# Attention's packed values contracted on 32x32 tiles of the PE array, with the exponentials turned by VectorE in place of TensorE

## The reference

```python
def sm_attn(qq, kk, vv):
    s = scale * np.matmul(qq, kk.transpose(0, 1, 3, 2))
    s = s - np.max(s, axis=-1, keepdims=True)
    a = np.exp(s)
    a = a / (np.sum(a, axis=-1, keepdims=True) + 1e-09)
    return np.matmul(a, vv)
p_packed = sm_attn(p, k, v)             # 32 packed rows against 576 keys
out = sm_attn(q, p_packed, p_packed)    # 576 tokens against 32 packed rows
# x: out as 4608 tokens x 512
xn = x / rms(x) * rms_g
x = (silu(xn @ w_gate) * (xn @ w_val)) @ w_out      # 512 -> 1536 -> 512
x = ((x @ w1) * (x @ w2) @ w3) @ w_out2             # 512 -> 1024 -> 1024 -> 512
```

## Time and profile before

| what | value |
|---|---|
| median of 3 runs | 1412.69 us |
| lowest and highest | 1411.97 and 1413.43 us |
| the profiled execution's own time | 1412.07 us |
| its span in the trace | 1410.3 us |
| PE busy, share of the span | 1386.3 us, 98% |
| DVE busy | 605.7 us, 43% |
| ACT busy | 406.9 us, 29% |
| POOL busy | 141.4 us, 10% |

### The profile page before, as it was taken

One profiled execution on the slowest core, in us unless ns is written; L12 is line 12 of the kernel. 1 busy time (PEld: TensorE's weight loads), 2 busy tenths in 40 slices (PEclk: granted clock), 3 DMA queues, 4 the chain that ended last, 5 costly groups with the idle time before them and its releaser, 6 DMA issues.

```text
span 1410.3 us, 22634 instructions
## 1 busy us (share of the span) xinstructions
PE 1386.3 (98%) x9688; PEld 1194.8 (85%) x9688; DVE 605.7 (43%) x1095; ACT 406.9 (29%) x803; POOL 141.4 (10%) x137
## 2 busy tenths in 40 slices
PE   7989999999999999999999999999999999999999
PEld 5679899898898998988989988888888888888887
DVE  3657556565565565655655632212212111212111
ACT  4253342433423424334233422111111111111111
POOL 0100100001001000010012030220202020202000
PEclk9999999999999999999999999999999999999999
DMA  9882451533424515323024130101011010100000
GB/s 332 233 314 82 129 163 41 196 106 93 165 86 128 163 39 197 107 92 131 18 69 167 47 107 0 60 0 60 0 60 45 16 60 0 60 0 30 0 30 30
DMA packets 59155, 129.13 MB, mean 92 GB/s; under 512 B 3504, under 2 KB 12720, under 8 KB 57264
## 3 DMA queue, kind: packets, MB, share of 16 engines
q1 hardware_dynamic: 59056, 127.70, 27.6%
HBM read 106.69 MB, written 20.99 MB: 91 GB/s over the span
## 4 chain that ended last, share of the span: by engine, by line
PE 95%; DVE 3%; ACT 1%; issue 1%; DMA 0%; SPq 0%; DVEq 0%; ACTq 0%
PE psum L586 9%; PE psum L584 9%; PE psum L585 9%; PE psum L546 8%; PE psum L565 7%; PE psum L567 7%; PE psum L566 7%; PE psum L547 7%; PE psum L548 7%; PE psum L606 5%; PE psum L605 5%; PE psum L604 5%; PE psum L513 3%; PE psum L500 1%; PE psum L526 1%; PE psum L467 1%
## 5 line engine op out<-in xcount | busy, mean ns | idle before, releaser
L546 PE MATMUL psum<-a_hi,m_hi 128*128 128x288 f32 x768 | 240.7, 313 | 0.4
L565 PE MATMUL psum<-g_hh,wo_hi 128*128 128x288 f32 x768 | 227.4, 296 | 4.5 <-DVE g_res L921 2.6
L547 PE MATMUL psum<-a_lo,m_hi 128*128 128x288 f32 x768 | 226.7, 295 | 0.0
L548 PE MATMUL psum<-a_hi,m_lo 128*128 128x288 f32 x768 | 226.3, 295 | 0.0
L567 PE MATMUL psum<-g_hh,wo_lo 128*128 128x288 f32 x768 | 226.0, 294 | 0.0
L566 PE MATMUL psum<-g_hl,wo_hi 128*128 128x288 f32 x768 | 225.9, 294 | 0.0
L1012 DVE TENSOR_TENSOR b_h<-b_s,psum 128x512 f32<-128x512 f32 x72 | 49.5, 688 | 408.9 <-PE psum L586 408.9
L584 PE MATMUL psum<-xh,w_hi 128*128 128x512 f32 x576 | 224.1, 389 | 0.0
L585 PE MATMUL psum<-xl,w_hi 128*128 128x512 f32 x576 | 224.1, 389 | 0.0
L586 PE MATMUL psum<-xh,w_lo 128*128 128x512 f32 x576 | 224.1, 389 | 0.0
L546 PEld LDWEIGHTS psum<-a_hi,m_hi 128*128 128x128 f32 x768 | 144.4, 188 | 50.6 <-issue 46.6
(11 more groups left out here) (109 smaller groups left out, 1737.2 us busy)
## 6 DMA issues: line engine op xcount, KB each, us to landing
w_in<-in_w_gate SPq DMA_DIRECT2D x24, 1024.0 KB, 5.3
w_in<-in_w_val SPq DMA_DIRECT2D x24, 1024.0 KB, 5.3
kT<-in_kT SPq DMA_DIRECT2D x8, 1152.0 KB, 7.7
v_sb<-in_v SPq DMA_DIRECT2D x8, 1152.0 KB, 7.2
qT<-in_qT SPq DMA_DIRECT2D x16, 576.0 KB, 3.8
y_scratch<-g_res SPq DMA_DIRECT2D x16, 576.0 KB, 3.2
x_raw<-y_scratch SPq DMA_DIRECT2D x9, 1024.0 KB, 7.6
out<-b_res SPq DMA_DIRECT2D x8, 1024.0 KB, 5.2
```

Source lines behind the costliest of these rows:

```text
L546: nc.tensor.matmul(in_ps[which], hi, a2_hi[:, t, par, :], start=par == 0, stop=False)
L547: nc.tensor.matmul(in_ps[which], hi, a2_lo[:, t, par, :], start=False, stop=False)
L548: last = nc.tensor.matmul(in_ps[which], lo, a2_hi[:, t, par, :], start=False, stop=par == 1)
L565: nc.tensor.matmul(out_ps[m], hi, hh[:], start=f == 0, stop=False)
```

## The change

The exponentials are no longer turned by TensorE. VectorE turns them in 32x32 blocks, from `sc` to the new tile `e1T` (`turn1`, one instruction for each parity): the block of head c's 32 packed rows and 32 keys stays on partitions 32 c to 32 c + 31, with the keys now on the partitions. The items AT and ScalarE's copies after them are gone, and so is `a1T`.

PV now contracts over 32 keys at a time: 18 blocks x 2 parities x 4 heads = 144 calls, weights 32 keys x 32 packed rows, moving operand 32 keys x 64 dimensions. The row tile of head (c, par) is c, and its column tile is `packed(par, c)`: c for even heads and c + 2 (modulo 4) for odd ones. So the packed rows of odd heads stand two places on in `pp`, in S2 and in M; `rden1` of odd heads is written by two reciprocals that move partitions, and `g` is laid out to match. `v` is laid out in 128 partitions in place of 96, with as many bytes. `sums1` moves from slot (0, 3) to (0, 5), and `turn1` stands in (0, 3) and (0, 4).

```diff
-SLOT_ITEM = {(0, 1): ("M", 0, 4), (0, 2): ("M", 0, 5), (0, 3): ("AT", 1, 0), (0, 4): ("AT", 1, 1), (0, 5): ("PV", 1, 0),
+SLOT_ITEM = {(0, 1): ("M", 0, 4), (0, 2): ("M", 0, 5), (0, 5): ("PV", 1, 0),
...
+def packed(par, c):
+    place = (c + 2 * par) % HC
+    return slice(NP * place, NP * (place + 1))
...
-            v_sb = at("v_sb", [TP, 2, NT, HC * DH])
+            v_sb = at("v_sb", [P, 2, NB, DH])
-            a1T = at("a1T", [TP, 2, NT * P])
+            e1T = at("e1T", [P, 2, S])
...
-                if kind == "AT":
-                    pe.wait_ge(e1_ready, 2 * a + part + 1)
-                    for j in range(NT):
-                        last = nc.tensor.transpose(xy[j // 3][0:TP, j % 3 * P:(j % 3 + 1) * P], sc[:, part, TP * j:TP * (j + 1)], ident[:])
                 if kind == "PV":
-                    freed(pe, "AT", a, 1)
+                    pe.wait_ge(e1T_ready, 2 * (a + 1))
                     pe.wait_ge(v_loaded, 16 * (a + 1))
-                    for par in range(2):
-                        for j in range(NT):
+                    for j in range(NB):
+                        for par in range(2):
                             for c in range(HC):
-                                last = nc.tensor.matmul(xy[par][NP * c:NP * (c + 1), 0:DH], a1T[:, par, P * j + NP * c:P * j + NP * (c + 1)],
-                                                        v_sb[:, par, j, DH * c:DH * (c + 1)], start=j == 0, stop=j == NT - 1)
+                                rows = slice(NP * c, NP * (c + 1))
+                                last = nc.tensor.matmul(xy[par][packed(par, c), 0:DH], e1T[rows, par, NP * j:NP * (j + 1)],
+                                                        v_sb[rows, par, j, :], start=j == 0, stop=j == NB - 1)
...
-                            rows, cols = slice(DH * par, DH * (par + 1)), slice(NP * c, NP * (c + 1))
+                            rows, cols = slice(DH * par, DH * (par + 1)), packed(par, c)
...
                 if kind == "S1":
                     full(act, "S1", a, part)
+                    if a:
+                        act.wait_ge(e1T_ready, 2 * a)
...
-                if kind == "AT":
-                    full(act, "AT", a, part)
-                    nc.scalar.copy(a1T[:, part, :].rearrange("p (a n) -> p a n", a=2), psum[0:TP, 6:8, 0:3 * P]).then_inc(xy_free, 1)
...
-                nc.vector.reciprocal(rden1[:], den1[:]).then_inc(rden1_ready, 1)
+                nc.vector.reciprocal(rden1[:, 0:1], den1[:, 0:1])
+                nc.vector.reciprocal(rden1[DH:P, 1:2], den1[0:DH, 1:2])
+                nc.vector.reciprocal(rden1[0:DH, 1:2], den1[DH:P, 1:2]).then_inc(rden1_ready, 1)
+
+            def turn1(a, par):
+                dve.wait_ge(e1_ready, 2 * a + par + 1)
+                if a:
+                    full(dve, "PV", a - 1, 0)
+                nc.vector.transpose(e1T[:, par, :], sc[:, par, :]).then_inc(e1T_ready, 1)
...
             fuse_split(0, 1)
+            turn1(0, 0)
+            turn1(0, 1)
             sums1(0)
...
-                        if b + 1 < B and (t, f) == (0, 3):
+                        if b + 1 < B and (t, f) in ((0, 3), (0, 4)):
+                            turn1(b + 1, f - 3)
+                        if b + 1 < B and (t, f) == (0, 5):
                             sums1(b + 1)
```

More of the change, by code:

```diff
@@ L41 @@
              (1, 8): ("M", 1, 2), (1, 9): ("M", 1, 3), (1, 10): ("S1", 2, 0), (1, 11): ("S1", 2, 1)}
-FIRST_ITEMS = [("S1", 0, 0), ("S1", 0, 1), ("AT", 0, 0), ("AT", 0, 1), ("PV", 0, 0), ("PT", 0, 0), ("S2", 0, 0), ("S2", 0, 1),
+FIRST_ITEMS = [("S1", 0, 0), ("S1", 0, 1), ("PV", 0, 0), ("PT", 0, 0), ("S2", 0, 0), ("S2", 0, 1),
                ("Z", 0, 0), ("Z", 0, 1), ("SS", 0, 0), ("M", 0, 0), ("M", 0, 1), ("M", 0, 2), ("M", 0, 3),
                ("S1", 1, 0), ("S1", 1, 1)]
+NB = S // NP
 W_BUFS = 4
@@ L126, in build @@
             raw = at("x_raw", [P, KC, TILE2])
-        const("first_region", [P, 22784])
+        const("first_region", [P, 22528])
         w3_hi, w3_raw, w3_lo = [None, None], [None, None], [None, None]
@@ L198, in build @@
         xy_full, xy_free = sem("xy_full"), sem("xy_free")
+        e1T_ready = sem("e1T_ready")
         nmax1_ready, bias1_ready, e1_ready = sem("nmax1_ready"), sem("bias1_ready"), sem("e1_ready")
@@ L614, in _ @@
             fuse(0, 1)
-            item("AT", 0, 0)
             fuse(0, 2)
-            item("AT", 0, 1)
             fuse(0, 3)
@@ L1038 @@
         "qT": q.transpose(0, 2, 4, 1, 3).reshape(B, P, HC, 2, HALF).transpose(0, 3, 1, 2, 4),
-        "v": v.reshape(B, HC, 2, NT, TP, DH).transpose(0, 4, 2, 3, 1, 5).reshape(B, TP, 2, NT, HC * DH),
+        "v": v.reshape(B, HC, 2, NB, NP, DH).transpose(0, 1, 4, 2, 3, 5).reshape(B, P, 2, NB, DH),
         "pT": p.transpose(0, 2, 4, 1, 3).reshape(B, P, HC * NP),
-        "g": np.asarray(inputs["moe_rms_g"]).reshape(KC, P).T,
+        "g": np.stack([np.asarray(inputs["moe_rms_g"]).reshape(HC, 2, DH)[(np.arange(HC) - 2 * par) % HC, par].T for par in range(2)]
+                      ).reshape(P, HC),
         "w_gate": inputs["moe_w_gate"], "w_val": inputs["moe_w_val"], "w_o": inputs["moe_w_out"],
```

## The result

The changed kernel takes 1450.7 us as a median of 4 runs (1449.5 to 1451.7), beside 1413.0 us (4 runs) for the kernel before: 1.027 times as long, with an interval of 1.0258 to 1.0282. I had predicted 1407.7 us, 5 us less. Its profiled execution took 1449.5 us, with a span of 1447.7 us where there were 1410.3.

The account below looks back on a forecast made before the run. TensorE's stream bounds the kernel (95% of the chain). AT's 1.31 us less PV's 0.67 gives 0.64 a batch, 5.1 over 8; less 0.2 stall, 4.9 off 1412.07; with 0.62 for the median, 1407.7 us, range 1405 to 1424.

Parts of the forecast that it names:

- PV grows: PV's item in each batch: 36 rounds of eight tiles plus ends, 2.33 us, 0.67 more than before.
- Rival C: TensorE's instructions run out in PV: 0.9 us more a batch, a loss of 2 us in all, 1415 us; chance 0.07.
- The clock: TensorE ahead of batch 0: the 3.4 us stretch at half clock may move or vanish, up to 1.7 us either way.
- Rival A: PV: only four tiles run at a time, 2.69 us more per batch, 1423.7 us in all; chance 0.10.
- rival B: PV's calls can't be issued faster than 28 ns each, 4.03 us an item, 1423.7 us in all; chance 0.11.
- the eight tiles side by side: PV's eight different tiles work at once, as S1's do: a round of 56 ns, 7.0 ns a record.
- The turning at 0.77 us: VectorE, slots (0, 3) and (0, 4): two turnings per batch at 0.78 us each, covered past the first batch.
- the stall in slot (0, 3) of batch 0: `outof` waits once for `g_hl` behind VectorE's turning: 0.15 to 0.45 us, taken as 0.2.
- the shift of odd heads: S2 and M keep eight tiles and their counts; the two extra reciprocals of 0.17 us make nobody wait.
- AT's worth: TensorE's stream: two AT items of 0.65 us go, 1.31 us a batch, 10.5 us over 8 batches.
- a hole inside PV in which nothing starts: Sign in PV's timeline of the changed profile, named for the case that instructions run out.

Follow-up runs that it names:

- e1T: Not a run: the changed kernel's new tile, into which VectorE turns the exponentials from `sc`; PV takes its weights from it.

## Why the prediction was wrong, point by point

**The step that failed** is "PV grows", in the sentence that sizes it: "36 rounds of 56 ns, 2.01 us, plus the same 0.32 at the ends". It asked what the array and the sequencer can do with instructions at hand, and took a burst of 16 calls for a run of 144. The item measures 5.1 to 10.1 us. Two terms make it up: the busy parts go at 9.9 ns a record in place of 7.0, 2.83 us in place of 2.01 (6.6 us over 8 batches), and the holes add 26.4 us.

**Rival C was the right mechanism with the wrong price and a chance of 0.07.** I had its 37 KB in 2 us and its 16 KB packets, but priced a packet by its transfer, 1.3 us. What counts is the time from one being used up to the next being usable: 3.5 us, measured with PV done twice. By that price 2.25 packets are 7.9 us, 4.9 more than AT and PV took before, so the rival would have reached up to 39 us of loss, 1452 us, less what is in stock: outside my range. The items measure 29 us of loss. The argument against it, "nothing waits on them, so a stock is likely", only showed that no run of the kernel before is long enough: 192 instructions in 1.55 us, with 48 in each 3.2 us step around. The section "Instruction fetch mechanics" of "Runtime: NRT & Kernel Launch" in the Trainium skill gives TensorE a store of 2048 instructions, though a note in it speaks of two lines of 16 KiB alone. The runs disagree with the 2048 and fit the two lines: in no batch of the changed kernel did more than 257 records, 514 instructions, pass before a hole. That is about two packets.

**The clock** I had as a matter of one stretch, worth 1.7 us either way. I missed that a hole can be followed by another: there are six such stretches, one where it was before and five behind holes, 27.3 us in all, up to 12 us of cost. Why the holes of three batches were followed by none stays open.

**Rival A** is refuted (14.1 ns on four tiles, 9.9 on eight), **rival B** as a price that each call always has, too (half of the calls cost 44 us less). What is left of B is the pace of 9.9 ns, just over the 9.2 at which I had the change break even: 0.32 + 2.83 = 3.15 us against 2.97. So even without any hole the change would have lost some 1.5 us, by this estimate. The Trainium skill's floor of 25 ns a matmul ("TensorE: Matmul & The Clock Gate", "Back-to-back issue gap") is not seen here either: two records of a call at 9.9 ns are 20 ns, and 17 ns with half of the columns.

**What held:** the eight tiles side by side, if not at 7 ns. The turning at 0.77 us, two per batch and free (1412.5 us alone), but for the stall in slot (0, 3) of batch 0 that I had at 0.2 us. It is there: from 105.18 to 105.67 are 0.49 us where two steps are 0.27, with `g_hl` ending at 105.37 (VectorE, then PE).

```profile
104.92 0.45 DVE L1008 TENSOR_TENSOR g_hl<-g_h,g_hh 128x288 fp32r<-128x288 f32 x1
105.18 0.29 PE L553 MATMUL psum<-a_hi,m_lo 128*128 128x288 f32 x1
105.43 0.41 PE L570 MATMUL psum<-g_hh,wo_hi 128*128 128x288 f32 x1
105.67 0.30 PE L571 MATMUL psum<-g_hl,wo_hi 128*128 128x288 f32 x1
```

 Nothing from the shift of odd heads. AT's worth, 0.65 us an item: seven items less gave 4.6 us (1412.6 to 1408.0), as worked out.

**Of the signs named ahead,** "a hole inside PV in which nothing starts" was the one that came.

## What to carry to other kernels

Count the instructions of a run, not only the array's time: here TensorE gets 256 instructions in 3.5 us, so a run of over 256 to 512 instructions that lasts less than 13.5 ns for each must be cut up or done with fewer and bigger ones, and small tiles buy nothing. Cutting it up needs room between the pieces: two pieces one step of 24 matmuls apart gave only half of the loss back. When a wait is put down to "issue", look for holes at a fixed distance in records and for a packet of the instruction queue ahead of each, and double or halve the run before believing in an engine's pace. Moving a turning from TensorE to an idle VectorE did pay (4.6 us, 0.3%), once the layout for the matmuls was kept; it stopped to pay as soon as the turnings filled the idle time ahead of the item.

## What was unexpected of the hardware

- TensorE's instructions come in packets of 256; by the records that pass before a hole (257 at most) two are at hand, and a third needs 3.45 to 3.73 us from one use to the next with the DMA queues idle (share 0.02). Ahead of batch 0, where their share is 1.04, it took 6.2 us (holes end at 27.82 and 34.02):

```profile
24.94 1.62 PE L484 MATMUL psum<-v_sb,e1T 32*32 32x64 f32 x140
27.82 1.47 PE L484 MATMUL psum<-v_sb,e1T 32*32 32x64 f32 x128 [1.27 <-issue]
34.02 0.64 PE L484 MATMUL psum<-v_sb,e1T 32*32 32x64 f32 x20 [4.72 <-issue]
```
```profile
24.00:36.00 12.00, 6.01 (x296) 4.83 (x295) 0.24 (x1) 1.30 (x4) 0.00 (x0) 0.86 1.04 386
```

  With PV done twice the same place has four holes, which end at 27.55, 33.74, 40.21 and 43.66 us: 6.2 and 6.5 us apart while the share is 1.05, and 3.45 once it falls:

```profile
33.70:40.20 6.50, 2.04 (x128) 1.81 (x128) 0.00 (x0) 0.00 (x0) 0.00 (x0) 0.50 1.05 385
40.20:43.70 3.50, 2.08 (x133) 1.85 (x135) 0.00 (x0) 0.00 (x0) 0.00 (x0) 0.50 0.49 180
```

  The packets themselves take 0.9 to 1.1 us each time; what grows is the time from the end of a hole to the start of the next packet, 3.8 us under load against 1.0 to 1.2 in the middle batches. That the loads in the queues cause this is argued from such places alone; it was not tried by itself.
- Waits of some 2 us or more in the middle of a busy stream were followed in five of eight batches by 3.4 or 6.8 us at half the clock, and 3.4 us of it cost 1.7, nearly as much again as a hole.
- A turning of 32 partitions x 192 columns to other partitions takes 0.37 us, where a third of the columns of the 0.78 us one would suggest 0.26.
